# The start of a convolution and two feed-forward layers: warm-up matmuls, table load, tile 1's input and ScalarE's second high part re-ordered

## The chip, the cores and the metric

One core of a Trainium2 chip. The time is that of one launch in device microseconds (us); the median of the runs shown is the figure that the prediction is about.

## The reference, cut to what matters

```python
x = causal_conv(x, softmax(weight))   # (4, 4096, 192), 7 taps, one softmax row per head of 24 channels
h = x @ w_in                          # 16384 x 192 by 192 x 2048
x = (h * cos(h)) @ w_out              # back to 16384 x 192
h = x @ w_in2
out = (h * clip(h + 3, 0, 6) / 6) @ w_out2
```

## The kernel before, in words

The 16384 tokens are cut into 32 tiles of 512. Channels lie on partitions: 128 of them in a main part, 64 in a tail. Each tile goes through layer 1 (L1, with the cosine) and layer 2 (L2, with the clip). A layer of a tile is a **phase** of 8 **slots**, and a slot makes two chunks (halves) of 128 hidden channels. The phases run L1 of tile 0, L1 of tile 1, L2 of tile 0, L1 of tile 2, L2 of tile 1 and so on, 64 phases and 512 slots in all; slots are numbered from 0 here. The first three phases are called setup 0 (slots 0 to 7), setup 1 (8 to 15) and setup 2 (16 to 23).

Every fp32 operand is split in a high part (fp32r, a rounding copy) and a low part (the difference), and products of high by high, high by low and low by high are summed. Two independent streams of matmuls use the upper and the lower 64 rows of the array at once (`lower` and `upper`, L520 and L539). A slot has 19 turns, one matmul of each stream in a turn: 9 first products each into `h_ps` (L450), and 10 second products (L457, L464) of the slot three before it. The first three slots have nothing to mix and run 14 turns, filled up with `unread` matmuls (`alone`, L572).

What one half of a slot goes through in L1: TensorE makes `h_ps`; ScalarE copies it to an integer (L692); VectorE subtracts (`fraction`, L821); ScalarE takes the cosine (L702); VectorE multiplies (`gated`, L832), which frees the half of `h_ps` for the slot after next (the wait at L501); ScalarE copies the high part `g_hi` (`high_part`, L704); GpSimd subtracts the low part `g_lo` (L1057). In L2 ScalarE does one Relu (L694) and VectorE one operation (L835) in place of the four. Every engine executes its list in the order in which it is written, so what stands behind a wait waits too.

Beside the slots, in an order written by hand:

- **Weights** come in 18 pieces. SyncE loads them (`load_piece`, L393); the stage buffer of a piece is reloaded when the low part of the piece before it in that buffer is done (L415). The high part is copied by ScalarE (L735) or VectorE (`weight_high`, L921; which slot, HIGH_BY_DVE in L268), the low part by GpSimd (`weight_low`, L1060; LOW_IN in L273 says before which slot's g_lo).
- **Input.** A tile's four main blocks and two tail blocks are loaded by SyncE (L379 to L391), tile 2's right behind piece 11 (L413), and VectorE transposes them (`turn_main` L866, `turn_x` L871, the latter in the last slot of a phase).
- **Convolution.** VectorE does the seven taps of the main part and, from tile 2 on, of the tail, one instruction for a tap. For tiles 0 and 1 the sum of the main part is kept in PSUM (`conv_first`, L912), and TensorE does both tails with f32 matmuls by diagonals (`convolve_tails`, L655). From tile 2 on the sums are in SBUF (`conv_taps`, L926). How many taps are done by the end of which slot is in the tables of L282 to L285.

Before slot 0, TensorE warms up on ones (L649), spreads the taps over the partitions (L431), warms up again and convolves the tails; ScalarE loads the exponential table with the softmax (L780), then the sine table (L782), makes the seven diagonals, and copies the high parts of weight pieces 0 to 3, of the input, and of pieces 4 and 5 (L787 to L796). `phase` of each engine runs the slots.

## Time and profile before

| | |
|---|---|
| runs (3) | 2240.67, 2240.82, 2241.79 us; median 2240.82 |
| the profiled execution's own time | 2242.02 us |
| its span, first to last instruction | 2240.3 us |
| PE, PEld, DVE, ACT, POOL busy | 99%, 82%, 81%, 77%, 67% of the span |
| granted TensorE clock over the span | 1.00 |

The span is 1.7 us under the execution's own time. Busy shares are averages; the start differs from the rest, so the start is read by itself. Slots are told apart by the one matmul in each that reads `in_twin` (L450), the fifth of the lower stream; it starts 0.9 us behind the slot's first matmul (four turns).

### The profile page before, as it was taken

The numbers are of one execution on the slowest core, as the hardware profiler recorded it, in microseconds if no ns is written. First come the engines' busy times: TensorE is split into PE (matmuls) and PEld (weight loads), VectorE is DVE, ScalarE is ACT, GpSimd is POOL, SyncE is SP. The second block draws the span as 40 slices with busy tenths as digits, with TensorE's granted clock in tenths as the row PEclk, the third lists the DMA queues.
The fourth block names the chain that finished last, engine by engine and source line by source line (L and its number), as shares of the span: only waits on it lengthen the run. The fifth ranks groups of instructions, "written<-read, shape, count | busy, mean of one in ns | idle before, by whom it ended". The sixth has DMA issues, their size and how long they took to land.

```text
span 2240.3 us, 56720 instructions
## 1 busy us (share of the span) xinstructions
PE 2227.1 (99%) x19519; PEld 1839.8 (82%) x19519; DVE 1824.4 (81%) x2503; ACT 1732.5 (77%) x2836; POOL 1511.3 (67%) x1067
## 2 busy tenths in 40 slices
PE   8999999999999999999999999999999999999999
PEld 6888888888888888888888888888888888888887
DVE  7878888888888888888888888888888888888754
ACT  6887777887777877778777788777787777877775
POOL 6976676666666666666666666666666666666664
PEclk9999999999999999999999999999999999999999
DMA  4100000000000000000000000000000000000001
GB/s 106 50 14 16 15 0 14 14 14 14 8 6 14 14 14 14 0 14 14 14 14 1 13 14 14 14 8 6 14 14 14 14 0 14 14 14 7 3 6 23
DMA packets 208556, 33.14 MB, mean 15 GB/s; under 512 B 203136, under 2 KB 207232, under 8 KB 208512
## 3 DMA queue, kind: packets, MB, share of 16 engines
q1 hardware_dynamic: 205872, 32.20, 8.2%
q8 instruction: 30, 0.49, 0.1%
q10 hardware_dynamic: 2640, 0.33, 0.1%
q14 instruction: 14, 0.11, 0.0%
HBM read 19.92 MB, written 12.58 MB: 15 GB/s over the span
## 4 chain that ended last, share of the span: by engine, by line
PE 96%; DVE 2%; ACT 1%; issue 0%; ACTq 0%; DVEq 0%
PE h_ps L450 45%; PE acc L457 30%; PE acc_tail L464 20%; DVE gate L832 1%; ACT pre L702 1%; DVE pre L821 0%; ACT g_hi L709 0%; PE acc_tail L661 0%; ACT pre L692 0%; DVE wout L924 0%; DVE acc L909 0%; DVE in_tail L945 0%; ACT in_tail L727 0%; DVE wtail_hi L924 0%; PE acc_tail L653 0%
## 5 line engine op out<-in xcount | busy, mean ns | idle before, releaser
L1057 POOL TENSOR_TENSOR g_lo<-gate,g_hi 128x512 fp32r<-128x512 f32 x1024 | 1471.5, 1457 | 709.2 <-ACT g_hi L709 706.8
L457 PE MATMUL acc<-g_hi,wout 64*128 64x512 f32 x4096 | 1416.1, 386 | 0.0
L457 PEld LDWEIGHTS acc<-g_hi,wout 64*128 64x128 f32 x4096 | 752.9, 184 | 79.0
L450 PE MATMUL h_ps<-in_hi,win_hi 64*128 64x512 f32 x2048 | 791.7, 387 | 6.1 <-DVE gate L832 6.0
L464 PE MATMUL acc_tail<-g_lo,wout 64*128 64x512 f32 x2048 | 791.5, 386 | 0.0
L464 PE MATMUL acc_tail<-g_hi,wout 64*128 64x512 f32 x2048 | 790.8, 386 | 0.0
L450 PE MATMUL h_ps<-in_tail,wtail_hi 64*128 64x512 f32 x2048 | 790.3, 386 | 0.5 <-DVE in_tail L945 0.5
L450 PE MATMUL h_ps<-in_lo,win_hi 64*128 64x512 f32 x2048 | 790.5, 386 | 0.0
L457 PE MATMUL acc<-g_lo,wout 64*128 64x512 f32 x2048 | 790.3, 386 | 0.0
L450 PE MATMUL h_ps<-in_hi,win_lo 64*128 64x512 f32 x2048 | 790.2, 386 | 0.0
L709 ACT ACTIVATE g_hi<-gate 128x512 fp32r<-128x512 f32 x1024 | 622.4, 631 | 115.2 <-DVE gate L835 54.3
L694 ACT ACTIVATE pre<-h_ps,three 128x512 f32<-128x512 f32 x512 | 347.7, 685 | 255.9 <-PE h_ps L450 255.9
L835 DVE SCALAR_TENSOR_TENSOR gate<-pre,h_ps 128x512 f32<-128x512 f32 x512 | 338.8, 680 | 178.0 <-ACT pre L694 164.9
L821 DVE TENSOR_TENSOR pre<-pre,h_ps 128x512 f32<-128x512 int32 x512 | 338.6, 686 | 147.7 <-ACT pre L692 143.0
L450 PEld LDWEIGHTS h_ps<-in_hi,win_hi 64*128 64x128 f32 x2048 | 376.8, 184 | 51.4 <-DVE gate L832 7.6
L450 PEld LDWEIGHTS h_ps<-in_tail,wtail_hi 64*128 64x128 f32 x2048 | 376.8, 184 | 40.7 <-DVE in_tail L945 0.9
L464 PEld LDWEIGHTS acc_tail<-g_hi,wout 64*128 64x128 f32 x2048 | 376.8, 184 | 40.0 <-issue 0.3
L464 PEld LDWEIGHTS acc_tail<-g_lo,wout 64*128 64x128 f32 x2048 | 376.8, 184 | 39.7
L450 PEld LDWEIGHTS h_ps<-in_hi,win_lo 64*128 64x128 f32 x2048 | 376.9, 184 | 39.4
L457 PEld LDWEIGHTS acc<-g_lo,wout 64*128 64x128 f32 x2048 | 376.7, 184 | 39.5
L450 PEld LDWEIGHTS h_ps<-in_lo,win_hi 64*128 64x128 f32 x2048 | 376.6, 184 | 39.5
L702 ACT ACTIVATE pre<-pre,half_pi 128x512 f32<-128x512 f32 x512 | 353.4, 720 | 64.0 <-DVE pre L821 50.9
(109 smaller groups left out, 2344.9 us busy)
## 6 DMA issues: line engine op xcount, KB each, us to landing
out_dram<-o_blk SPq DMA_DIRECT2D x128, 64.0 KB, 1.8
x_in<-in_x SPq DMA_DIRECT2D x127, 64.0 KB, 2.2
blk_tail<-in_x SPq DMA_DIRECT2D x62, 64.0 KB, 2.2
out_dram<-blk_tail SPq DMA_DIRECT2D x62, 64.0 KB, 1.8
stage<-in_moe_w_out SPq DMA_DIRECT2D x7, 384.0 KB, 3.3
stage<-in_moe_w_in SPq DMA_DIRECT2D x3, 512.0 KB, 4.0
stage<-in_moe_w_in SPq DMA_DIRECT2D x6, 256.0 KB, 4.0
pre<-in_moe_w_in SPq DMA_DIRECT2D x2, 256.0 KB, 4.3
```

The source lines that it names most:

```text
L450: return pe.matmul(chunk_of(h_ps, q, half), w, x, start=start, stop=stop)
L457: return pe.matmul(acc[pair][:, :], wout[layer][rows, 2 * q + half, cols], g[rows, :], start=start, stop=stop)
L464: return pe.matmul(acc_tail[pair][:, :], wout[layer][rows, 2 * q + half, P:2 * P], g[rows, :], start=start, stop=stop)
L694: i = act.activation(p, h, ACT.Relu, bias=three[:, 0:1])
L702: act.activation(p, p, ACT.Sin, bias=half_pi[:, 0:1], scale=-TWO_PI).then_inc(cos_ready, 1)
L709: act.activation(chunk_of(g_hi, q, half), chunk_of(gate, q, half), ACT.Copy).then_inc(ghi_ready, 1)
L821: dve.tensor_tensor(p, p.bitcast(I32), chunk_of(h_ps, q, half), ALU.subtract).then_inc(frac_ready, 1)
L832: dve.tensor_tensor(g, p, h, ALU.mult).then_inc(g_ready, 1)
L835: dve.scalar_tensor_tensor(out=g, in0=p, scalar=6.0, in1=h, op0=ALU.min, op1=ALU.mult).then_inc(g_ready, 1)
L1057: pool.tensor_tensor(chunk_of(g_lo, q, half), chunk_of(gate, q, half), chunk_of(g_hi, q, half).bitcast(F32), ALU.subtract).then_inc(glo_re ...
```

## The change

- TensorE's warm-up: 5 pairs of fp32r matmuls (64 rows, 512 columns, both row halves) in place of 7 f32 ones of 128 columns; behind the spreading of the taps 3 pairs in place of 3.
- ScalarE loads the exponential table at once, with an unused activation, and then issues two main blocks (in place of one) and the two tail blocks of tile 0. Weight piece 3's high part goes behind `split_hi`.
- SyncE loads tile 1's main blocks behind pieces 0 and 1, once `xT` has been written, in place of behind piece 6.
- VectorE transposes tile 1, keeps its halo and does three of its seven taps before slot 0. In setup 0 one tap is left in slots 1 and 2 each and two in slot 3; the high parts of pieces 8 and 9, and the low tail, move by a slot.
- In setup 1 no tap of tile 2 is done; `put_halo` and all 14 taps go to setup 2, slots 16 to 20, three a slot but two in slot 19. Before, four were done in setup 1 and ten in setup 2.
- ScalarE, in setup 0 and 1: the second half's `g_hi` goes behind the two copies of the next slot.
- GpSimd's low parts of pieces 8 to 14 go one slot later.

```diff
 LAG = 3
-WARM_BEFORE = 7
+WARM_BEFORE = 5
 WARM_BEHIND = 3
...
         three = sb("three", [P, 1])
-        unused = sb("unused", [P, 1])
+        unused = sb("unused", [P, 2])
         w_soft = sb("w_soft", [H, TAPS])
...
         OUT_PIECES = {0: [5, 7, 8, 9], 2: [14, 15, 16, 17]}
-        HIGH_BY_DVE = {0: {0: 6, 1: 7, 2: 8, 4: 9, 6: 10}, 1: {0: 11, 2: 12, 4: 13, 6: 14}}
+        HIGH_BY_DVE = {0: {0: 6, 1: 7, 3: 8, 5: 9, 6: 10}, 1: {0: 11, 2: 12, 4: 13, 6: 14}}
         HIGH_IN = {2: {0: 15, 2: 16, 4: 17}}
...
         LOW_FIRST = 6
-        LOW_IN = {1: 6, 2: 7, 3: 8, 5: 9, 7: 10, 9: 11, 11: 12, 13: 13, 15: 14, 18: 15, 20: 16, 22: 17}
+        LOW_IN = {1: 6, 2: 7, 4: 8, 6: 9, 8: 10, 10: 11, 12: 12, 14: 13, 16: 14, 18: 15, 20: 16, 22: 17}
...
         LAST_TURN = DRAIN_SLOT + 1
-        CONV_FIRST = [0, 0, 1, 3, 5, 7, 7, 7, 7]
-        TURN_1 = 0
-        CONV_SECOND = [0, 0, 1, 2, 2, 2, 2, 3, 4]
+        CONV_BEFORE = 3
+        CONV_FIRST = [3, 3, 4, 5, 7, 7, 7, 7, 7]
+        CONV_SECOND = [0, 0, 0, 0, 0, 0, 0, 0, 0]
+        CONV_THIRD = [0, 3, 6, 9, 11, 14, 14, 14, 14]
         CONV = {0: [0, 0, 0, 1, 1, 1, 2, 3, 4], 1: [4, 6, 8, 10, 11, 14, 14, 14, 14]}
-        TWIN_1, TAIL_1, LOW_TAIL_1, HIGH_1, LOW_1 = 1, 3, 4, 5, 5
+        TWIN_1, TAIL_1, LOW_TAIL_1, HIGH_1, LOW_1 = 1, 2, 3, 4, 5
         LAST_LOWER = [(0, MAIN, 6), (0, TAIL, 4), (1, TAIL, 4), (1, MAIN, 6), (2, TAIL, 4), (2, MAIN, 6)]
...
-            done = {0: CONV_FIRST, 1: CONV_SECOND}.get(ph.setup, CONV[ph.layer])
+            done = {0: CONV_FIRST, 1: CONV_SECOND, 2: CONV_THIRD}.get(ph.setup, CONV[ph.layer])
             return range(done[q], done[q + 1])
...
             sp.dma_start(w_soft[:, :], weight).then_inc(w_loaded, 16)
-            load_main(0, range(P // BLK - 1))
+            load_main(0, range(2))
             for b in range(P // BLK, BLOCKS_D):
                 sp.dma_start(chip_block(x_in, o_blk_tail, b), dram_block(x_blocks, 1, b)).then_inc(x_tail_loaded, 16)
-            for n in range(LOADED_FIRST):
+            for n in range(2):
                 load_piece(n)
...
             load_main(1, range(P // BLK))
+            for n in range(2, LOADED_FIRST):
+                load_piece(n)
             for n in range(LOADED_FIRST, len(PIECES)):
...
-                ones = in_f[L2][:, 0:P]
+                ones = in_hi[L1]
                 for _ in range(count):
-                    pe.matmul(acc_tail[0][:, 0:P], ones, ones, start=True, stop=True)
+                    for rows, n in ((LOW, 0), (UP, 1)):
+                        pe.matmul(chunk_of(h_ps, n, 1), ones[rows, 0:P], ones[rows, :], start=True, stop=True)
...
-            def high_part(q, slot, reused):
+            def high_half(q, slot, half):
+                act.wait_ge(g_ready, 2 * slot + half + 1)
+                act.activation(chunk_of(g_hi, q, half), chunk_of(gate, q, half), ACT.Copy).then_inc(ghi_ready, 1)
+
+            def high_part(q, slot, reused, halves):
                 if reused:
                     act.wait_ge(mix_done, slot - G_BUFS + 1)
-                for half in range(2):
-                    act.wait_ge(g_ready, 2 * slot + half + 1)
-                    act.activation(chunk_of(g_hi, q, half), chunk_of(gate, q, half),
-                                   ACT.Copy).then_inc(ghi_ready, 1)
+                for half in range(halves):
+                    high_half(q, slot, half)
...
                         act.wait_ge(wlo_done, 2 * q + 2)
+                    if ph.setup == 2 and q == 0:
+                        high_half(SLOTS - 1, slot - 1, 1)
                     before_gate(ph.layer, q, slot)
+                    if ph.setup in (0, 1) and slot > 0:
+                        high_half((q - 1) % SLOTS, slot - 1, 1)
                     if ph.layer == L1:
...
                         split_high(L2, L1)
-                    high_part(q, slot, ph.setup != 0 or q >= G_BUFS)
+                    high_part(q, slot, ph.setup != 0 or q >= G_BUFS, 1 if ph.setup in (0, 1) else 2)
                     if splits_next(ph, q):
...
-            act.dma_start(chip_block(x_in, x_in_tail, P // BLK - 1),
-                          dram_block(x_blocks, 0, P // BLK - 1)).then_inc(x_loaded, 16)
+            act.wait_ge(const_ready, 1)
+            act.activation(unused[:, 1:2], half_pi[:, :], ACT.Exp)
+            for b in range(2, P // BLK):
+                act.dma_start(chip_block(x_in, x_in_tail, b), dram_block(x_blocks, 0, b)).then_inc(x_loaded, 16)
             for b in range(P // BLK, BLOCKS_D):
...
             act.wait_ge(const_ready, CONSTS)
-            act.activation(unused[:, :], half_pi[:, :], ACT.Sin)
+            act.activation(unused[:, 0:1], half_pi[:, :], ACT.Sin)
             act.wait_ge(taps_ready, 2)
...
                 act.activation(diagonal(t), eye, ACT.Copy, scale=taps[:, TAIL, t:t + 1]).then_inc(diag_ready, 1)
-            for n in range(4):
+            for n in range(3):
                 weight_high(n)
...
             split_hi(acc[0][:, :], L2)
+            weight_high(3)
             act.wait_ge(tails_convolved, 1)
...
                                       in_twin[L1][DT:P, :].bitcast(F32), ALU.subtract).then_inc(lo_ready[L1], 1)
-                    keep_halo(1)
                 if q == LOW_1:
...
                     if ph.convolved is not None:
-                        if ph.layer == L1 and ph.setup != 0 and q == 0:
+                        if q == 0 and (ph.setup == 2 or ph.layer == L1 and ph.setup not in (0, 1)):
                             put_halo(ph.convolved)
...
                     if ph.setup == 0:
-                        if q == TURN_1:
-                            turn_main(1)
                         split_low_1(q)
...
-            dve.memset(in_f[L2][:, 0:P], 1.0).then_inc(ones_ready, 1)
+            dve.memset(in_hi[L1][:, :].bitcast(F32), 1.0).then_inc(ones_ready, 1)
             dve.memset(half_pi[:, :], HALF_PI).then_inc(const_ready, 1)
...
                 conv_first(0, t)
-            split_low_main(acc[0][:, :], L2, 0)
-            split_low_tail(acc_tail[1][0:DT, :], L2, 0)
             keep_halo(0)
             dve.wait_ge(halo_ready, 4)
+            turn_main(1)
+            split_low_main(acc[0][:, :], L2, 0)
+            split_low_tail(acc_tail[1][0:DT, :], L2, 0)
+            keep_halo(1)
+            for t in range(CONV_BEFORE):
+                conv_first(1, t)
             phase(first_phase())
```

## Rows read from the trace of the kernel before

**Rows 1.** The page, parts 1 and 5: busy time, and the costliest group.
```profile
PE 2227.1 (99%) x19519; PEld 1839.8 (82%) x19519; DVE 1824.4 (81%) x2503; ACT 1732.5 (77%) x2836; POOL 1511.3 (67%) x1067
...
L1057 POOL TENSOR_TENSOR g_lo<-gate,g_hi 128x512 fp32r<-128x512 f32 x1024 | 1471.5, 1457 | 709.2 <-ACT g_hi L709 706.8
```

**Rows 2.** Busy time of the instructions that touch in_twin, 500 to 930.67 us.
```profile
500.00:930.67 430.67, 38.60 (x100) 18.40 (x100) 0.00 (x0) 7.58 (x12) 1.00 0.07 11
```

**Rows 3.** PE in order of time: start, us, line, tiles [idle <-releaser].
```profile
27.77 0.39 PE L450 MATMUL h_ps<-in_twin,wtail_lo 64*128 64x512 f32 x1
...
49.00 0.49 PE L450 MATMUL h_ps<-in_hi,win_hi 64*128 64x512 f32 x1 [2.65 <-DVE gate L832]
...
59.05 0.39 PE L450 MATMUL h_ps<-in_twin,wtail_lo 64*128 64x512 f32 x1
...
80.58 0.39 PE L450 MATMUL h_ps<-in_twin,wtail_lo 64*128 64x512 f32 x1
...
96.09 0.38 PE L450 MATMUL h_ps<-in_twin,wtail_lo 64*128 64x512 f32 x1
```

**Rows 4.** DVE in order of time, 20 to 70 us.
```profile
33.44 0.99 DVE L924 CAST wout<-stage 128x768 fp32r<-128x768 f32 x1
...
46.71 1.29 DVE L821 TENSOR_TENSOR pre<-pre,h_ps 128x512 f32<-128x512 int32 x2
48.26 1.30 DVE L832 TENSOR_TENSOR gate<-pre,h_ps 128x512 f32<-128x512 f32 x2 [0.26 <-ACT pre L702]
...
58.15 0.71 DVE L869 STREAM_TRANSPOSE xT<-x_in 128x512 f32<-128x512 f32 x1
```

**Rows 5.** ACT in order of time, 42 to 49 us.
```profile
42.87 1.07 ACT L692 ACTIVATE pre<-h_ps 128x512 int32<-128x512 f32 x2
47.44 1.33 ACT L702 ACTIVATE pre<-pre,half_pi 128x512 f32<-128x512 f32 x2 [3.50 <-DVE pre L821]
```

**Rows 6.** PE in order of time, the f32 convolution of the tails.
```profile
7.12 5.04 PE L661 MATMUL acc_tail<-xT_tail,oT 128*128 128x512 f32 x8
...
12.00 2.74 PE L661 MATMUL acc_tail<-xT_tail,sum_tail 128*128 128x512 f32 x6
```

**Rows 7.** SP's queue in order of time, before and with tile 1's input; the last block alone.
```profile
7.97 0.43 SPq L395 DMA_DIRECT2D gate<-in_moe_w_out  x1
...
9.64 4.44 SPq L382 DMA_DIRECT2D x_in<-in_x  x4
...
12.21 1.87 SPq L382 DMA_DIRECT2D x_in<-in_x  x1
```

**Rows 8.** DMA issues of the kernel: count, KB each, median us to landing.
```profile
gate<-in_moe_w_out SPq DMA_DIRECT2D x1, 384.0 KB, 7.6
```

**Rows 9.** ACT in order of time, the last weight part before slot 0.
```profile
17.02 0.83 ACT L738 ACTIVATE wout<-gate 128x768 fp32r<-128x768 f32 x1
```

**Rows 10.** POOL in order of time, 45 to 48 us.
```profile
45.38 1.96 POOL L1068 TENSOR_TENSOR wout<-stage,wout 128x512 fp32r<-128x512 f32 x2
```

**Rows 11.** SP's queue in order of time, 47 to 53 us.
```profile
47.37 1.11 SPq L395 DMA_DIRECT2D stage<-in_moe_w_in  x2
48.52 2.18 SPq L382 DMA_DIRECT2D x_in<-in_x  x4
50.74 1.18 SPq L390 DMA_DIRECT2D blk_tail<-in_x  x2
```

**Rows 12.** L390 from 51.5 to 51.8 us: tile 2's last block, issue and landing.
```profile
L390 SPq DMA_DIRECT2D blk_tail<-in_x x1: 488/488/488, 51.4 to 51.4; - x1
...
DMA to landing us min/median/max: 2.3/2.3/2.3
```

**Rows 13.** DVE by line and shape: count, busy us, mean ns, idle.
```profile
L909 DVE SCALAR_TENSOR_TENSOR in_ftail<-xT_tail,taps,in_ftail 64x512 f32<-64x512 f32 x180 | 288.5, 1603 | 0.0
L909 DVE SCALAR_TENSOR_TENSOR in_f<-xT,taps,in_f 128x512 f32<-128x512 f32 x180 | 226.5, 1259 | 0.0
...
L909 DVE SCALAR_TENSOR_TENSOR acc<-xT,taps,acc 128x512 f32<-128x512 f32 x12 | 9.1, 754 | 0.3
```

More of the change, by code:

```diff
@@ L1032, in _ @@
                 conv_first(0, t)
+            keep_halo(0)
+            dve.wait_ge(halo_ready, 4)
+            turn_main(1)
             split_low_main(acc[0][:, :], L2, 0)
             split_low_tail(acc_tail[1][0:DT, :], L2, 0)
-            keep_halo(0)
-            dve.wait_ge(halo_ready, 4)
+            keep_halo(1)
+            for t in range(CONV_BEFORE):
+                conv_first(1, t)
             phase(first_phase())
```

## The prediction

> **What bounds the kernel now.** The page comes first: TensorE (PE) is busy 99% of the span and GpSimd (POOL) 67% [rows 1], so the steady part can't gain from this change, which touches only the start. Next the busy time by tile: 100 of the matmuls that read `in_twin`, one per slot, in 430.67 us, so a slot takes 4.307 us [rows 2] and a turn 0.227. With that pace the order of time on PE shows what the start wastes [rows 3]. From slot 3's marker at 27.77 to slot 9's at 59.05 are 31.28 us, where six slots need 25.84: 5.44 lost, half of it in one wait of 2.65 for VectorE's gate before slot 7. From slot 14's (80.58) to slot 17's (96.09) are 15.51 where three need 12.92: 2.59 lost. Between and behind these PE runs at its pace. So some 8 us can be had in the slots, besides what lies before slot 0.
>
> Why PE waits there: half 0 of a slot is ready 12 x 0.227 + 0.39 = 3.1 us after its first matmul and half 1 after 4.25. The slot after next needs the gate of half 0 at 8.61. In L1, VectorE (DVE) needs about 2.75 us of a slot for fraction and gate (1.29, a gap of 0.26, 1.30, less overlaps) [rows 4]. Anything over 1.55 us beside them becomes a backlog. In slot 4 of before there stand two taps, a weight part, the low tail and tile 1's halo copies; ScalarE (ACT) meanwhile waits 3.50 us for the fraction [rows 5].
>
> **Start.** The exponential table goes in front, but DVE's memset of the ones is four times as wide, and ACT issues a DMA more before the softmax; I count the two as equal. The diagonals' matmuls of the tails take 5.04 us for 8, then 2.74 for 6 [rows 6]: 0.63 and 0.46 each, so TensorE comes to its upper level (2.4 GHz) on the way. Whether fp32r pairs bring it there sooner no row shows. All 14 at 0.43 would end 1.5 us sooner than 14.6, all at the lower level's 0.85 some 4.4 us later. A gain there is hidden: ACT makes the last weight part, piece 5, at 17.02 to 17.85 [rows 9], just before it copies slot 0's first half, and piece 5 lands 7.6 us after its issue [rows 8] at 7.97 [rows 7]. SyncE (SP) now issues tile 1's four blocks ahead of pieces 2 to 6. At 9.64 they took 4.44 us of SP's queue, the last alone 1.87 [rows 7]; tile 2's four took 2.18 [rows 11]. I take the nearest to the latter, 2.1 us, as few bytes are in flight then: pieces 2 to 6 are issued 2 us later, piece 5 lands at 17.6, ACT is through with it at 18.4. **+0.2** us for slot 0; ends -0.6 (the clock, no delay) and +5.6 (each block held up for 1.87, which is 5.4 more, piece 2 holding ACT's split as well). Turning tile 1 and three taps (0.71 + 3 x 0.75 [rows 4, 13]) lie in DVE's idle time before slot 0.
>
> **Setup 0.** ACT now copies the next slot before the second g_hi, about 0.55 us sooner for DVE. I walk through the slots with the durations of rows 4 and 5, from an unchanged gate 0. The turn (0.71) is out of slot 0, so gate 1 and with it slot 3 come 0.8 us sooner: at 26.0 in place of 26.8 (27.77 less four turns). Slots 1 and 2 have a tap each and piece 7: gates 2 and 3 are there at 30.25 and 34.55, in time for slots 4 and 5 (30.3, 34.6). Behind gate 3, slot 3 has two taps (1.5), piece 8 (0.99) and the low tail (0.7, as half of the 1.30 of two gates): DVE is free at 38.2, fraction to gate half 0 takes 1.55 + 0.67, so gate 4 is there at 40.4 where slot 6 is due at 38.95: **1.5 us stall**. Slot 4 has nothing beside it; slots 7, 8 and 9 start in time, at 44.8, 49.1 and 53.4. Slot 9 started at 59.05 - 0.9 = 58.15: **-4.75** us (0.8 + 5.44 - 1.5). The ends are -5.5 and -3.5 (piece 8 or 9 held up once more by as much as the 1.3 of a second POOL operation would be).
>
> **What is late next: tile 2's input.** DVE turns tile 2 in slot 7. SP loads it behind piece 11, which waits for piece 9's low part on POOL. Before: that part ends at 47.34 [rows 10], SP issues piece 11 at 47.37, the tail blocks end their issue at 51.9 [rows 11], the last one starts at 51.43 and lands 2.3 us later [rows 12]: at 53.7, 6.4 us after the low part, 4.4 us before DVE's turn at 58.15 [rows 4]. Now that low part goes a slot later, behind g_lo of slot 5 whose second half goes behind ACT's copies of slot 6: copies end 46.4, g_hi 47.0, g_lo 48.35, low part 50.3. The input is there at 56.7, DVE comes for it at 52.7. After the two transposes (57.3), fraction and gate of slot 8 end at 59.5; slot 10 is due at 57.7: **+1.85**. Ends 0 and +2.5.
>
> **Setup 1.** Here ACT splits tile 0's layer-2 input between slots 12 and 13, and DVE's weight parts remain; four taps are gone, and the copies come 0.55 sooner, against the first of the three gaps before slots 15, 16 and 17. By the same walk gate 13 is early for slot 15. The low tail, from SBUF like the slow taps, and piece 14 still cost some 0.4 at slots 16 and 17. 2.59 - 0.4: **-2.2**; ends -2.6 (all of it) and -1.2 (the 0.55 alone at each gap, and some of the taps).
>
> **Setup 2.** The fourteen taps of tile 2 now stand in slots 16 to 20. A tap that sums in SBUF has a mean of 1.26 (main) and 1.60 us (tail), one in PSUM 0.754 [rows 13]. The trace shows no other difference than POOL's work beside it, and POOL is full in these slots. Three taps are about 4.2 us, two 2.5, the gate 1.3, the drain of slot 19 another 1.3: DVE has 5.5, 5.5, 5.1 and 5.5 us in slots 17 to 20 against PE's 4.3. That is a backlog of 4.4 us; by the walk DVE comes in with some 2.3 to spare, so slots 21, 22 and 23 wait 0.2, 0.7 and 1.2: **+2.1**. Ends 0 (taps at 0.754, as in PSUM: 3.6 us a slot) and +3.8 (all at 1.60).
>
> The Trainium skill (SBUF — State Buffer, section Who interferes with whom) says that a VectorE instruction with two SBUF inputs contends with a GpSimd instruction that reads SBUF, and that the one that comes second blocks until the first ends. That speaks against the move from setup 1 to setup 2: by it, the twelve two-input taps could each wait out a whole g_lo. The means of rows 13 agree that such taps cost more, so far by half to a whole microsecond. Its worst case is a rival below.
>
> **The sum.** +0.2 - 4.75 + 1.85 - 2.2 + 2.1 = -2.8 us. The profiled execution took 2242.02 with a span of 2240.3; it would be 2239.2 and 2237.5. It stands 1.2 us over the median, so the median goes from 2240.82 to 2238.0. What a measurement of this kernel can tell from no change is about 0.2%, 4.5 us: faster means under 2236.3, slower over 2245.3.
>
> **Rivals.**
> - As summed, both new waits there: 0.48, 2238.0, its own range 2236.8 to 2239.6.
> - One of the two is absorbed (tile 2's blocks early enough, or DVE's slack in setup 2 enough): 0.20, 2236.0. For it: the slack of 4.4 us at DVE's turn before; against: the low part is a slot later.
> - Both absorbed: 0.08, 2234.1.
> - The change doesn't do what it says: g_hi's second half behind the copies feeds POOL late, so that PE waits for g_lo in slots with a low weight part. The slack that I find is 3.2 us, and such a part takes 1.96 [rows 10]; with a second delay of a POOL operation (1.457 [rows 1]) it is 0.2 to 0.4 over. Seven such slots at 0.35 give back 2.4: 0.14, 2240.4.
> - **Slower:** weights behind tile 1's blocks. If SP is held up 1.87 us at each block, piece 2 is issued 7.5 us later, ACT stands before it with `split_hi` behind, and slot 0 comes 5.6 us later in place of 0.2, with the rest as summed: 2238.0 + 5.4 = 2243.4. It decides once piece 5 lands after some 17.4 (18.2 less 0.83 [rows 9]). For it the 1.87 [rows 7], against it the 2.18 for four [rows 11] and the little in flight at 5.6 us. 0.08.
> - Each two-input tap waits out a whole POOL operation (1.457 [rows 1]): 12 x (0.75 + 1.46) = 26.5 us against my 17.8, so 8 more: 2246. 0.02. The page on SBUF named above gives the rule; the means of rows 13 are well under it.
>
> **How the numbers follow.** The range from 2234.6 to 2241.0 takes in the first four but half of the third, and leaves out the last two. Faster by over 0.2%: half of the second case, the third and a little of the first, 0.23. Slower: the last and the far end of the fifth, 0.03. Within: 0.74.
>
> **What would show it.** In the changed kernel: slot 9's marker near 54.3, slot 7 without a wait; a gap of about 1.5 us before slot 6 and of 1.9 before slot 10, there with DVE waiting for `x_in` in slot 7; no gap before slot 15; gaps before slots 21 to 23 with VectorE's taps behind one another; slot 24's marker 2.8 us earlier than before, and from there an even pace. Piece 5 landed by 17.6 and slot 0's first copy near 18.4. The forecast is wrong if slot 0's copy comes over 1 us off, if the turn of tile 2 finds its input, or if PE waits for POOL anywhere.

## The result and the profile after

| | before | after |
|---|---|---|
| median of the runs | 2241.76 us (13 runs, 2240.14 to 2242.34) | 2246.32 us (13 runs, 2245.12 to 2247.24) |
| ratio to before, 95% interval | | 1.002 [1.0012, 1.0029] |
| profiled execution's own time, span | 2242.02, 2240.3 us | 2246.53, 2244.8 us |
| granted TensorE clock over the span | 1.00 | 0.999 |

The changed kernel is 4.6 us slower, where 2.8 us less were forecast; the time lies outside the range, and the interval is clear of 1. The forecast was wrong, at two of its five terms. One run of experiment 8 took 4254.20 us at a granted clock of 0.52 over its whole span, and its ratio leaves that run out.

The slots are read by the same marker as before, the matmul that reads `in_twin`. PE in order of time in the kernel after (start, us, engine, line, operation, tiles): slots 0, 9, 10, 11, 14, 17 and 24.

```profile
19.24 0.39 PE L453 MATMUL h_ps<-in_twin,wtail_lo 64*128 64x512 f32 x1
...
57.40 0.39 PE L453 MATMUL h_ps<-in_twin,wtail_lo 64*128 64x512 f32 x1
...
65.64 0.62 PE L453 MATMUL h_ps<-in_twin,wtail_lo 64*128 64x512 f32 x1
...
71.30 0.39 PE L453 MATMUL h_ps<-in_twin,wtail_lo 64*128 64x512 f32 x1
...
84.22 0.39 PE L453 MATMUL h_ps<-in_twin,wtail_lo 64*128 64x512 f32 x1
...
97.69 0.39 PE L453 MATMUL h_ps<-in_twin,wtail_lo 64*128 64x512 f32 x1
...
130.77 0.39 PE L453 MATMUL h_ps<-in_twin,wtail_lo 64*128 64x512 f32 x1
```

Slots 9, 14 and 17 stood at 59.05, 80.58 and 96.09 before [rows 3], slot 0 at 16.48 and slot 24 at 126.26. From slot 24 on the two traces run 4.5 us apart to the end (4.51 at slot 24 and at the last slot), at the pace of [rows 2]. So all of the difference lies ahead of slot 24:

| stretch | forecast | measured (after less before) |
|---|---|---|
| before slot 0 | +0.2 | 19.24 - 16.48 = +2.76 |
| slots 0 to 9 | -4.75 | 38.16 - 42.57 = -4.41 |
| slots 9 to 11, tile 2's input late | +1.85 | 13.90 - 8.61 = +5.29 |
| slots 11 to 18 | -2.2 | -2.06 |
| slots 18 to 24 | +2.1 | +2.93 |
| sum | -2.8 | +4.51 |

**Before slot 0.** VectorE in order of time; last the reason of its wait:

```profile
7.96 0.71 DVE L893 STREAM_TRANSPOSE xT_tail<-blk_tail 128x512 f32<-128x512 f32 x1 [1.91 <-DMA blk_tail<-in_x]
```

TensorE in order of time, the f32 convolution of the tails behind that transpose:

```profile
8.73 6.20 PE L665 MATMUL acc_tail<-xT_tail,oT 128*128 128x512 f32 x8 [1.38 <-DVE xT_tail L893]
14.77 2.74 PE L665 MATMUL acc_tail<-xT_tail,sum_tail 128*128 128x512 f32 x6
```

Before, the eight began at 7.12 and took 5.04 [rows 6]. Now they begin 1.61 us later, behind a wait of 1.38, and take 1.16 more, since more of them ran at the lower clock level (a matmul each 0.85 us in place of 0.43). Together that is the difference of 2.76, to rounding. The second part scatters: in the five profiles that have this start the eight took 5.31 to 6.67, in the nine others 4.72 to 6.10, so 1.16 is this pair's number and not the change's alone. The weights are not the cause: SP's queue in order of time (start, us from first issue to the end of the last) shows tile 1's four blocks in 1.91 us, and ScalarE reached piece 5 with slot 0 already running.

```profile
5.59 1.91 SPq L383 DMA_DIRECT2D x_in<-in_x  x4
```

ScalarE in order of time, the last weight part of the start [rows 9 before: 17.02]:

```profile
19.78 0.83 ACT L744 ACTIVATE wout<-gate 128x768 fp32r<-128x768 f32 x1
```

**Slots 9 to 11.** GpSimd, SyncE, VectorE, ScalarE and TensorE in order of time: piece 9's low part, tile 2's issues, their consumer, and who stands behind it.

```profile
51.04 2.44 POOL L1082 TENSOR_TENSOR wout<-stage,wout 128x512 fp32r<-128x512 f32 x2
...
54.67 2.18 SPq L383 DMA_DIRECT2D x_in<-in_x  x4
56.89 2.41 SPq L391 DMA_DIRECT2D blk_tail<-in_x  x2
...
60.10 0.71 DVE L882 STREAM_TRANSPOSE xT<-x_in 128x512 f32<-128x512 f32 x1 [4.45 <-DMA x_in<-in_x]
61.44 0.70 DVE L888 STREAM_TRANSPOSE xT_tail<-blk_tail 64x512 f32<-64x512 f32 x1 [0.62 <-DMA blk_tail<-in_x]
...
62.75 1.33 ACT L706 ACTIVATE pre<-pre,half_pi 128x512 f32<-128x512 f32 x2 [5.12 <-DVE pre L834]
...
64.32 0.50 PE L453 MATMUL h_ps<-in_hi,win_hi 64*128 64x512 f32 x1 [3.31 <-DVE gate L845]
```

Read it downwards: the low part ends at 53.5 where it ended at 47.34 before [rows 10], the issues start at 54.67 where they started at 48.52 [rows 11], VectorE waits 4.45 and 0.62 where it came to data already there [rows 4], and behind it the cosine and then TensorE wait. TensorE's own wait isn't the whole loss. Busy time of the engines by stretch (stretch, length, busy us and count of PE, PEld, DVE, ACT, POOL, granted clock, DMA share, GB/s):

```profile
60.00:65.00 5.00, 1.69 (x16) 1.18 (x14) 4.01 (x7) 1.98 (x4) 1.34 (x1) 1.00 0.39 118
65.00:68.40 3.40, 3.40 (x20) 2.65 (x18) 2.97 (x5) 3.12 (x6) 2.74 (x2) 0.50 0.00 0
68.40:72.00 3.60, 3.60 (x34) 2.93 (x34) 1.47 (x3) 2.45 (x6) 1.74 (x2) 1.00 0.01 2
```

TensorE was busy 1.69 us of the five, and then the granted clock stood at 0.50, the lower level of 1.2 GHz, for 3.4 us: 20 matmuls, where the next line has 34. The loss of 5.29 is 3.5 us of lateness (slot 10's first matmul at 64.32, where 57.40 - 0.9 + 4.31 = 60.81 was due), and about half of 3.4 us for the clock.

**Slots 18 to 24.** VectorE in order of time: tile 2's halo and some of its taps.

```profile
99.92 1.27 DVE L908 COPY xT_tail<-halo_tail 64x6 f32<-64x6 f32 x1
...
106.03 1.77 DVE L922 SCALAR_TENSOR_TENSOR in_f<-xT,taps,in_f 128x512 f32<-128x512 f32 x1
107.73 1.78 DVE L922 SCALAR_TENSOR_TENSOR in_ftail<-xT_tail,taps,in_ftail 64x512 f32<-64x512 f32 x1
```

The four steps from slot 19 to 23 took 4.95, 5.73, 4.75 and 4.72 in place of 4.31. The pair of taps shown, beside POOL's work, took 3.5 us, and a copy of six columns, which takes 0.16 elsewhere, took 1.27.

### The profile page after: what moved, and what is told of

Read it like the earlier page. It is cut to its first block, busy times and chain, and to the rows that moved or that the text cites. A ratio compares the mean times of both kernels' runs of the same rounds, so it can differ in the third digit from the quotient of the medians.

```text
span 2244.8 us, 56713 instructions
## 1 busy us (share of the span) xinstructions
PE 2229.0 (99%) x19515; PEld 1837.4 (82%) x19515; DVE 1825.9 (81%) x2503; ACT 1729.7 (77%) x2837; POOL 1509.3 (67%) x1067
## 4 chain that ended last, share of the span: by engine, by line
PE 95%; DVE 2%; ACT 2%; DMA 0%; issue 0%; SPq 0%; POOL 0%; ACTq 0%; DVEq 0%; POOLq 0%
PE h_ps L453 45%; PE acc L460 30%; PE acc_tail L467 20%; ACT g_hi L710 1%; DVE gate L845 0%; PE acc_tail L665 0%; ACT pre L706 0%; DMA blk_tail<-in_x 0%; ACT pre L696 0%; ACT pre L698 0%; DVE pre L834 0%; DVE gate L848 0%; DVE in_f L922 0%; DVE wout L937 0%; POOL g_lo L1071 0%
## 5 line engine op out<-in xcount | busy, mean ns | idle before, releaser
L453 PEld LDWEIGHTS h_ps<-in_hi,win_hi 64*128 64x128 f32 x2048 | 377.1, 184 | 51.8 <-DVE gate L845 5.3
```

Of the source, the lines that this page charges most:

```text
L453: return pe.matmul(chunk_of(h_ps, q, half), w, x, start=start, stop=stop)
```

## The experiments

Most start from the changed kernel. A marker is the start of the `in_twin` matmul of a slot; "slot 0 to 24" is the time between two of them, which leaves out what lies before slot 0, and "slot 6 takes 4.63" is the time from slot 5's marker to slot 6's. Numbers 1 to 5 ran once each, so only their traces are argued from; their times are given for scale (the kernel before, beside the first four, took 2241.94).

**1. The start as before** (`e_start`).

```diff
-            load_main(0, range(2))
+            load_main(0, range(P // BLK - 1))
...
-            act.wait_ge(const_ready, 1)
-            act.activation(unused[:, 1:2], half_pi[:, :], ACT.Exp)
-            for b in range(2, P // BLK):
+            for b in range(P // BLK - 1, P // BLK):
```

> The changed kernel, but SyncE again issues three of tile 0's main blocks and ScalarE one and the two tail blocks, without the early exponential table. Theory A (the start is late because tile 0's last tail block, issued third on ScalarE's queue at 3.1 us, lands at 7.87 behind weight piece 0): the tail block lands by 5 us, VectorE's wait of 1.9 us for it goes, slot 0's in_twin matmul comes at 16.5 to 17.2 in place of 19.24, and slot 24's is 2 to 2.8 us earlier than in the changed kernel. Theory B (slot 0 is late because pieces 2 to 5 come behind tile 1's blocks): the tail block comes earlier, but slot 0 stays over 18.5 and slot 24 moves by under 1 us. The wait for tile 2's input stays in both.

Measured: 2243.92 us; slot 0 at 16.96, 2.3 us earlier than in the kernel after. The stall before slot 10 stays (8.35 from slot 9 to 10). So putting back the order of issue and taking out the early table wins back about 2.3 of the 2.8 us (number 10 shows that they don't cost it alone), and the start isn't why tile 2's input is late.

**2. Tile 2's input ahead of piece 9, in place of behind piece 11** (`e_x2`). The number in the edit is that of a piece and not of a slot: SyncE issues the input from 30.89 us on, in place of 54.67. Where an expectation below says that it is loaded in slot 9, this is meant.

```diff
-                if n == 12:
+                if n == 9:
                     load_x(2)
```

> The changed kernel, but SyncE loads tile 2's input ahead of piece 9 in place of behind piece 11. Theory A (the wait of 4.45 us before the turn of tile 2 costs 3.9 us at slot 10, and the fall of TensorE's clock that follows the gap 1.4 more): the step from slot 9's to slot 10's in_twin matmul falls from 8.23 to 4.3 us and the next from 5.66 to 4.3, the granted clock is 1.00 there, and slot 24's comes 4.5 to 5.3 us earlier. Rival (VectorE's backlog or GpSimd's late low parts would hold slot 10 anyway, the input is only what shows): the steps stay over 5 us, and slot 24 moves by under 3 us.

Measured: 2240.85 us, 5.5 less than the median after. Slots 10 and 11 run at the pace, and the granted clock is 1.00 there. TensorE in order of time, slots 10 and 11 of this kernel:

```profile
61.20 0.39 PE L453 MATMUL h_ps<-in_twin,wtail_lo 64*128 64x512 f32 x1
...
65.50 0.39 PE L453 MATMUL h_ps<-in_twin,wtail_lo 64*128 64x512 f32 x1
```

This one number (12 to 9) is worth the whole 5.3 us of slots 9 to 11: with the wait gone, the fall of the clock is gone too.

**3. Four taps back in setup 1** (`e_taps`).

```diff
-        CONV_SECOND = [0, 0, 0, 0, 0, 0, 0, 0, 0]
-        CONV_THIRD = [0, 3, 6, 9, 11, 14, 14, 14, 14]
+        CONV_SECOND = [0, 0, 1, 2, 2, 2, 2, 3, 4]
...
-                        if q == 0 and (ph.setup == 2 or ph.layer == L1 and ph.setup not in (0, 1)):
+                        if ph.layer == L1 and ph.setup != 0 and q == 0:
```

> The changed kernel, but four of tile 2's fourteen taps are done in slots 8 to 15 again and ten in 16 to 23. Theory A (three taps a slot put VectorE over TensorE's pace in slots 17 to 20, which costs 2.93 us at slots 20 to 23): the steps from slot 19 to 24 are all 4.3 us, slots 15 to 17 lose at most 1 us more than the 0.57 they lose in the changed kernel, so slot 24 comes 1.9 to 2.9 us earlier. Rival (the moved taps cost the same wherever they stand): slots 15 to 17 lose as much as is won, slot 24 moves by under 1 us.

Measured: 2245.36 us. Slots 20 to 24 are even at 4.31, so setup 2's loss is the moved taps' doing. But slots 16 and 17 take 5.00 and 5.91: slot 24 stands at 129.49, only 1.3 us earlier than after. The move costs 2.9 us in setup 2 and saves 1.74 in setup 1. So slot 24 moved by less than the theory had (1.9 to 2.9) and by a little more than the rival (under 1).

**4. Both high parts at once** (`e_ghi`), without the deferral of the second one.

```diff
-                    if ph.setup == 2 and q == 0:
-                        high_half(SLOTS - 1, slot - 1, 1)
...
-                    if ph.setup in (0, 1) and slot > 0:
-                        high_half((q - 1) % SLOTS, slot - 1, 1)
...
-                    high_part(q, slot, ph.setup != 0 or q >= G_BUFS, 1 if ph.setup in (0, 1) else 2)
+                    high_part(q, slot, ph.setup != 0 or q >= G_BUFS, 2)
```

> The changed kernel, but ScalarE copies both high parts of a slot before the next slot's copies, as before the change. Theory A (the reorder gives VectorE about 0.5 us a slot and so slots 3 to 9 some 1 to 2.5 us, and makes tile 2's load late by about 1 us, as piece 9's low part on GpSimd stands behind the deferred half): slots 3 to 9 lose 1 to 2.5 us more, the wait for tile 2's input is 1 to 3 us shorter, slot 11 is within 1.5 us of the changed kernel's; slots 15 to 17 lose 0.5 to 1.5 us more. Rival (the deferred half is what makes the input late): slot 11 comes 3 us or more earlier.

Measured: 2248.45 us, of which 1.0 is this execution's later start (slot 0 at 20.28: the tail block landed at 8.44 and the eight matmuls took 6.67). From slot 0 to 24 it took 112.35 against 111.53 after, and from slot 0 to 9, ahead of the stall, 38.83 against 38.16. So the deferral is worth 0.67 us there, under the 1 to 2.5 expected. The stall before slot 10 blurs the rest, so the comparison was made again in number 9.

**5. Piece 9 a slot sooner** (`e_low9`), high part in slot 4 and low part ahead of slot 5, as tile 2's input waits behind it.

```diff
-        HIGH_BY_DVE = {0: {0: 6, 1: 7, 3: 8, 5: 9, 6: 10}, 1: {0: 11, 2: 12, 4: 13, 6: 14}}
-        LOW_IN = {1: 6, 2: 7, 4: 8, 6: 9, 8: 10, 10: 11, 12: 12, 14: 13, 16: 14, 18: 15, 20: 16, 22: 17}
+        HIGH_BY_DVE = {0: {0: 6, 1: 7, 3: 8, 4: 9, 6: 10}, 1: {0: 11, 2: 12, 4: 13, 6: 14}}
+        LOW_IN = {1: 6, 2: 7, 4: 8, 5: 9, 8: 10, 10: 11, 12: 12, 14: 13, 16: 14, 18: 15, 20: 16, 22: 17}
```

> The changed kernel, but piece 9 as before the change: high part in slot 4, low part on GpSimd ahead of slot 5's g_lo. Theory A (tile 2's load waits for that low part, which went a slot later, and the order of the loads is what costs): SyncE issues piece 11 at 48.5 to 50 in place of 53.5, tile 2's last block lands by 57, VectorE waits under 1 us for it in place of 5.1, slots 10 and 11 lose nothing to 0.6 us, the granted clock stays 1.00, and slot 24 comes 4 to 5.5 us earlier. Rival (it is the deferred half of g_hi that makes the low part late, the slot matters little): piece 11 is still issued after 51.5 and slot 10's step stays over 6 us.

Measured: 2241.16 us, slot 24 at 125.28, 5.5 us earlier. VectorE comes to tile 2 without a wait, and SP has the issues out by 53.8. VectorE, then SyncE, of this kernel in order of time:

```profile
55.03 0.70 DVE L882 STREAM_TRANSPOSE xT<-x_in 128x512 f32<-128x512 f32 x1
...
50.38 2.18 SPq L383 DMA_DIRECT2D x_in<-in_x  x4
52.60 1.24 SPq L391 DMA_DIRECT2D blk_tail<-in_x  x2
```

So the chain of the forecast is the right one: low part of piece 9, piece 11, tile 2's blocks, VectorE. The two tail issues take 1.24 here, and 2.41 in the kernel after.

**6. Numbers 1 and 2 together** (`e_both`).

> Both single edits at once: tile 0's input issued as before the change (SyncE three main blocks, ScalarE one and the tails, no early table) and tile 2's input loaded ahead of piece 9. Theory A (the two losses are separate: 2.3 us at the start and 5.3 at slots 10 and 11): slot 0's in_twin matmul at 16.5 to 17.2, slot 10 and 11 at even steps, slot 24's at 122 to 123.5; the time is 7 to 8 us under the changed kernel, 2238.0 to 2239.5, faster than before the change by 2 to 4 us. Rival (what comes earlier at the start only waits later, for weights): 2240 to 2242, with new steps over 4.5 us in slots 3 to 9.

Measured: 2238.44 us median (11 runs, 2237.87 to 2239.81) against 2241.88 of the kernel before beside it (27 runs), ratio 0.9987 [0.9978, 0.9996]. Its profile is of its fastest execution (2237.87). Slot 0 at 16.29, slot 24 at 122.07, 8.7 earlier than after: 2.95 before slot 0, 5.29 in slots 9 to 11, 0.46 elsewhere. With the two failed terms taken out, the rest of the change is a gain of 3.4 us.

**7. The warm-up alone, on the kernel before** (`b_warm`).

```diff
-WARM_BEFORE = 7
+WARM_BEFORE = 5
...
-                ones = in_f[L2][:, 0:P]
+                ones = in_hi[L1]
...
-                    pe.matmul(acc_tail[0][:, 0:P], ones, ones, start=True, stop=True)
+                    for rows, n in ((LOW, 0), (UP, 1)):
+                        pe.matmul(chunk_of(h_ps, n, 1), ones[rows, 0:P], ones[rows, :], start=True, stop=True)
...
-            dve.memset(in_f[L2][:, 0:P], 1.0).then_inc(ones_ready, 1)
+            dve.memset(in_hi[L1][:, :].bitcast(F32), 1.0).then_inc(ones_ready, 1)
```

> The kernel before with the new warm-up alone: 5 and 3 pairs of fp32r matmuls of 512 columns in place of 7 and 3 f32 ones of 128. Theory A (the warm-up changes nothing that counts: in all traces so far TensorE stays at its lower level until some 10 to 15 us, long after it): within 0.5 us of before, slot 0's matmul at 16 to 17.5, the diagonals' matmuls still start at spaces of 0.85 us. Rival (the pairs bring the upper level sooner): those matmuls start at spaces of 0.43 from the first and the time is 0.7 to 1.5 us under before. Third (pairs of half the rows count as less activity, the level rises later): 0.7 us or more over before.

Measured: 2242.59 us (11 runs), ratio 1.0005 [0.9996, 1.0014]; slot 0 at 16.35 against 16.48. The pairs make no difference at slot 0 and none in the time that is clear of noise. The median is 0.7 us above the kernel before, though, outside the 0.5 of theory A and at the edge of the third rival. That rival's reason isn't what the trace shows: the eight matmuls of the tails took 4.78 us in place of 5.04, and what this profile loses, it loses at slot 8 (5.92 in place of 4.70), behind a fall of the clock.

**8. Four taps in slots 8 to 10** (`e_spread`): number 6, with ten taps left for setup 2.

```diff
-        CONV_SECOND = [0, 0, 0, 0, 0, 0, 0, 0, 0]
-        CONV_THIRD = [0, 3, 6, 9, 11, 14, 14, 14, 14]
+        CONV_SECOND = [0, 1, 3, 4, 4, 4, 4, 4, 4]
...
-                        if q == 0 and (ph.setup == 2 or ph.layer == L1 and ph.setup not in (0, 1)):
+                        if ph.layer == L1 and ph.setup != 0 and q == 0:
```

> The kernel with both edits, and the taps of tile 2 split anew: four in slots 8 to 10 (one, two, one), where VectorE has only a weight part or nothing beside the gates, ten in slots 16 to 20. Theory A (a tap is free where VectorE stays under TensorE's 4.31 us a slot, and costs where it goes over): steps from 19 to 24 all 4.3, the steps of 8 to 15 all 4.3, 16 as in the changed kernel; 2.5 to 3 us under the kernel with both edits, 2235 to 2237. Rival (a tap costs GpSimd or VectorE the same anywhere): within 1 us of it.

Measured: 2240.56 us median (11 runs, 2240.09 to 2241.66 and the one of 4254.20), ratio 0.9994 [0.9985, 1.0004], 2.1 slower than number 6. Slots 20 to 24 are even, but slots 11, 13, 15 and 16 take 6.24, 5.63, 5.45 and 5.25. Both the theory and the rival missed. What the expectation had left out is the halo: VectorE in order of time, one of its two copies of six columns, which took 1.83 and 1.26. They stand ahead of the loss at slot 11; whether they also bring the losses at slots 13 to 16 isn't shown.

```profile
57.96 1.83 DVE L905 COPY xT<-halo 128x6 f32<-128x6 f32 x1
```

**9. Number 6 without the deferral** (`e_noghi`), the edit of number 4.

> e_both without the later second high part (ScalarE makes it ahead of the next copies, as in the kernel before). Theory (the deferral pays a little in every setup slot): slots 3 to 9 take 0.7 to 1.5 us more than in e_both and slots 15 and 16 0.6 more; 0.8 to 2 us above e_both's 2238.4, so 2239.2 to 2240.4. Rival (it only moves waits): within 0.5 us of e_both.

Measured: 2240.89 us median (10 runs), ratio to before 0.9998 [0.9989, 1.0007], 2.45 above number 6. Both start within 0.04 us of one another; slots 0 to 9 take 39.23 against 37.67, and slots 15 and 16 5.15 and 5.24 against 4.31 and 4.84. By the medians the deferral is worth 2.5 us, a little more than the theory's upper end (2.46 against number 11, which has the deferral too). Of the 1.56 us in slots 0 to 9 some 0.5 is luck of number 6's profile: there VectorE's copy of weight piece 6 took 0.69 us, and slots 3 and 4 are even; in number 11, with the same list for these slots, the copy took 1.80 and slots 0 to 9 38.19. Number 6, then number 11:

```profile
21.94 0.69 DVE L935 CAST wtail_hi<-stage 128x1024 fp32r<-128x1024 f32 x1
```

```profile
21.96 1.80 DVE L937 CAST wtail_hi<-stage 128x1024 fp32r<-128x1024 f32 x1
```

**10. The order of issue alone, on the kernel before** (`b_issue`).

```diff
-            load_main(0, range(P // BLK - 1))
+            load_main(0, range(2))
...
+            act.wait_ge(const_ready, 1)
+            act.activation(unused[:, 1:2], half_pi[:, :], ACT.Exp)
+            for b in range(2, P // BLK):
```

> The kernel before with only the start's new order of issue: the exponential table first, and tile 0's two tail blocks third and fourth on ScalarE's queue in place of second on their own; warm-up, tile 1's load, taps and high parts as before. Theory (the late tail block costs the start 2 to 3 us): tile 0's last tail block lands at 7 to 8 us, the first twin group stands at 18.5 to 19.5 us in place of 16.48, and the time is 2.0 to 2.8 us above the kernel before. Rival (the block lands late only because tile 1's blocks are issued beside it): first twin group within 0.5 us of 16.48 and no change of the time.

Measured: 2241.11 us median (10 runs), ratio 0.9997 [0.9988, 1.0007], slot 0 at 16.30. My theory fell: the last tail block is third and fourth in line here too, and it is early. L780 of this kernel, the issues of tile 0's tail blocks, with DMA from issue to landing (min, median, max):

```profile
L780 ACTq DMA_DIRECT2D blk_tail<-in_x x2: 510/510/510, 2.1 to 2.7; - x2
...
DMA to landing us min/median/max: 2.5/2.6/2.6
```

The same issues in the kernel after, L790:

```profile
L790 ACTq DMA_DIRECT2D blk_tail<-in_x x2: 511/511/511, 2.5 to 3.1; - x2
...
DMA to landing us min/median/max: 2.7/3.7/4.8
```

There the last block is issued 0.43 us later, at 3.09, with SP's issue of weight piece 0 at 3.26, and takes 4.8 us in place of 2.6. This is no single case: in all five profiles of kernels in which it is issued at 3.1 it took 4.8 to 5.5 us, and in the nine in which it is issued by 2.7 it took 2.8 at most. That it waits for the weight piece behind it is likely and not shown; no run moved that piece alone. What puts it later is another edit: the memset of the ones, four times as wide for the new warm-up (0.48 us in place of 0.17), stands ahead of the memset of `half_pi`, for which ScalarE waits before the table, and its four DMA issues with it. Neither edit alone moves slot 0 later (numbers 7 and 10). That is a new theory, so it got a run.

**11. `half_pi` ahead of the ones** (`e_memset`): number 2 and two lines exchanged.

```diff
+            dve.memset(half_pi[:, :], HALF_PI).then_inc(const_ready, 1)
             dve.memset(in_hi[L1][:, :].bitcast(F32), 1.0).then_inc(ones_ready, 1)
-            dve.memset(half_pi[:, :], HALF_PI).then_inc(const_ready, 1)
```

> The changed kernel with tile 2's input loaded in slot 9 (e_x2), and besides the memset of half_pi ahead of the memset of the ones. Only the start differs from e_x2. Theory (the wide memset holds back the exponential table's wait, and with it ScalarE's four DMA issues, by 0.4 us; the last tail block is then issued 0.17 us ahead of weight piece 0 and lands with it): that block is issued near 2.65 and lands before 5.8 us, the first twin group stands 1.5 to 2.8 us earlier than e_x2's 18.81, at 16.0 to 17.3, and the time is 2238.0 to 2239.4 in place of 2240.85. Rival (issued third and fourth on ScalarE's queue, with tile 1's blocks behind it, it lands late anyway): the block still lands after 7.5 us and the time stays within 0.5 us of 2240.85.

Measured: 2238.43 us median (10 runs), ratio to before 0.9987 [0.9977, 0.9996]; 2.4 less than number 2's one run, and equal to number 6, which undoes the order of issue and the early table. L790 of this kernel:

```profile
L790 ACTq DMA_DIRECT2D blk_tail<-in_x x2: 511/511/511, 1.9 to 2.5; - x2
...
DMA to landing us min/median/max: 2.5/2.5/2.6
```

Its first marker:

```profile
16.32 0.39 PE L453 MATMUL h_ps<-in_twin,wtail_lo 64*128 64x512 f32 x1
```

So 2.5 us at slot 0 hang on whether a memset of 0.48 us stands ahead of one of 0.06.

**12. A version that beats both** (`e_best`): number 6, with tile 2's halo put in slot 9 and the low tail of setup 0 and 1 a slot later.

```diff
-        TWIN_1, TAIL_1, LOW_TAIL_1, HIGH_1, LOW_1 = 1, 2, 3, 4, 5
+        TWIN_1, TAIL_1, LOW_TAIL_1, HIGH_1, LOW_1 = 1, 2, 4, 4, 5
...
-                        if q == 0 and (ph.setup == 2 or ph.layer == L1 and ph.setup not in (0, 1)):
+                        if ph.layer == L1 and ph.setup != 0 and q == (1 if ph.setup == 1 else 0):
```

> e_both with tile 2's halo put in slot 9 in place of slot 16, and the low tail steps of the setup one slot later (position 4 in place of 3). Theory (the stalls of e_both before slots 6 and 20 to 23 come from the work that is put into those slots, on DVE's queue): the step to slot 6, 5.85 us in e_both, comes down to about 5.1, and the 2.9 us that slots 20 to 23 lose in e_both come down to about 1; 1.5 to 2.5 us faster than e_both's 2238.4, so 2235.8 to 2237.5. Rival (GpSimd's operations block DVE's taps in slots 20 to 23 whatever else stands there): slots 20 to 23 keep their stalls, at most 0.7 us faster, 2237.7 to 2238.6.

Measured: 2236.57 us median (11 runs, 2235.91 to 2237.44), ratio to before 0.9979 [0.997, 0.9988], 1.9 less than number 6 and 9.75 less than the kernel after. Slot 6 takes 4.63 in place of 5.86 (5.49 in number 11), though slots 3 and 4 take 0.8 more; number 11 has these 0.8 too, so they aren't this edit's. Slot 20 is even, and slots 21 to 23 still lose 0.7, 0.4 and 0.4. From slot 0 to 24 it took 104.01 against 105.78. Theory and rival both have a part: the halo's copies are out of setup 2 (in slot 9, with no operation of POOL beside them, they take 0.16 each), and the taps that POOL holds up, at 1.77 to 1.84 each, stay.

## Why the prediction was wrong

**Start, +0.2: failed, +2.76.** The step that failed reads "I count the two as equal": the exponential table in front against the wider memset and the DMA more. I weighed them as work on VectorE and ScalarE, and not as what stands ahead of tile 0's last tail block. That block was issued at 3.09 in place of 1.77 and landed at 7.87 in place of 4.5, VectorE waited 1.91, and TensorE began the tails 1.61 later. Numbers 7, 10 and 11 show the cause: the two edits together, neither alone. The second part, 1.16 us, is time at the lower clock level, and it scatters from one execution to the next. The forecast named a cost from the lower level (up to 4.4 us if all 14 stayed there), but a second step failed: "A gain there is hidden", behind ScalarE's piece 5. The tails weren't hidden, not even in the kernel before. There ScalarE waited 1.96 us for them, and piece 5 was through at 17.85, with slot 0 already running, while the first copy of slot 0 waited 0.38 more for TensorE:

```profile
14.78 0.59 ACT L727 ACTIVATE in_tail<-acc_tail 64x512 fp32r<-64x512 f32 x1 [1.96 <-PE acc_tail L661]
...
18.22 0.60 ACT L692 ACTIVATE pre<-h_ps 128x512 int32<-128x512 f32 x1 [0.38 <-PE h_ps L450]
```

In the kernel after the wait for them is 2.34 us:

```profile
17.55 0.59 ACT L733 ACTIVATE in_tail<-acc_tail 64x512 fp32r<-64x512 f32 x1 [2.34 <-PE acc_tail L665]
```

So whatever delays the tails delays slot 0. The delay of the weights was read rightly in size: tile 1's four blocks took 1.91 for the 2.1 taken, and the slower rival (1.87 for each) did not come.

**Setup 0, -4.75: right, -4.41.** The wait of 2.65 before slot 7 is gone, slot 7 takes 4.31. The gap before slot 6 was 1.14 for a forecast of 1.5, with 0.45 before slot 4 besides. How much of the gain is the deferral's depends on the pair that is compared: 0.67 (number 4 and the kernel after), 1.04 (numbers 9 and 11), 1.56 (numbers 9 and 6).

**Tile 2's input, +1.85: the chain right, the term mis-sized, +5.29.** The forecast had VectorE there at 52.7 and the input at 56.7, a wait of 4.0. The start's delay moved both ends by 2.8: VectorE came at 55.65, the low part ended at 53.5 (50.3 + 2.8 + 0.4). Then 6.4 us had been allowed from there to the last landing, and it took 7.9 (61.42): a tail block's issue took 1.88 where both took 1.18 before [rows 11], and its landing 2.6 for 2.3 [rows 12]. That made TensorE's lateness 3.5 in place of 1.85, and the rest, 1.8, is the fall of the clock, which the sum did not have at all. Numbers 2 and 5 take the wait away in two ways, and each gains 5.3 in slots 9 to 11. The upper end of +2.5 was too low for both reasons.

**Setup 1, -2.2: right, -2.06.** Slots 15 and 17 are even; slot 16 takes 4.84, a loss of 0.53 for 0.4.

**Setup 2, +2.1: right, +2.93, by a walk that erred both ways.** The backlog came, within the bounds, but a slot sooner: slots 20 to 23 lose 0.64, 1.42, 0.44 and 0.41 where 0, 0.2, 0.7 and 1.2 were walked. What brought it forward is the halo's copy of 1.27, for which the term had nothing; number 12 moves it, makes slot 20 even and leaves a loss of 1.6. The taps themselves came out cheaper than the 1.48 used. The rival by which each two-input tap waits out a whole POOL operation gives 2246, near the result, but by coincidence: the twelve such taps took from 0.73 to 1.78, a mean of 1.34, far under the rival's 2.21. Some are held for most of an operation and some not at all.

The Trainium skill (SBUF — State Buffer, section Who interferes with whom) says that of a VectorE instruction with two SBUF inputs and a GpSimd instruction that reads SBUF the second blocks until the first ends. This trace is in line with that for single taps, 1.77 for 0.73, while the mean of 1.34 stays well under the worst case.

**The rivals.** The two by which a new wait is absorbed fell: both waits came. The slower one, by tile 1's blocks, didn't come, as said. GpSimd fed late (2240.4) fell with number 9, and with TensorE's waits in the kernel after, from 16 to 130 us (who waited for whom: us in total, times, the longest): no matmul waited for POOL. One weight load did, for 0.76 us ahead of slot 0, while TensorE was still at the tails.

```profile
PE h_ps L453 <- DVE gate L845: 4.6, 4, 3.3
PE h_ps L453 <- DVE gate L848: 1.5, 2, 1.1
PE h_ps L453 <- DVE in_tail L958: 0.5, 1, 0.5
```

Without the two failed terms the sum of the others as measured is -4.41 - 2.06 + 2.93 = -3.5, and number 6 came out at -3.4. What was wrong was not the plan of the slots, but the two places where DMAs and a memset feed it.

## What to carry to other kernels

When an edit puts a wait ahead of a queue's DMA issues, follow that wait to the instruction that releases it and to everything in front of that: 0.3 us of memset became 2.5 us at the first slot, and two edits, neither of which moved slot 0 alone, cost this together. A load's slack is counted at its consumer, with the worst issue and landing seen, and a wait of TensorE like the 3.3 us here is priced with the slow stretch that may follow it. And a start is best tried in pieces: of five terms three were right, and two lines (number 11) turned a loss of 4.6 us into a gain of 3.4.

## What the runs showed that I had not expected

- **The clock can fall behind a gap.** Behind TensorE's wait of 3.3 us the granted clock was 0.50 for 3.4 us. At the gap before slot 7, whose profile has a wait of 2.65 both in the kernel before and in number 7, it fell in one and not in the other. Busy time by stretch, number 7, then the kernel before:

```profile
50.00:54.00 4.00, 4.00 (x24) 3.18 (x22) 3.09 (x5) 3.35 (x7) 2.26 (x2) 0.57 0.78 122
```

```profile
50.00:54.00 4.00, 3.89 (x34) 2.92 (x32) 2.99 (x5) 3.35 (x7) 2.36 (x2) 1.00 0.82 130
```

  Nothing here tells what decides it; slot 8 took 5.92 in place of 4.70.
- **The start scatters.** Numbers 6 and 12 have the same code before slot 0, and the eight f32 matmuls took 4.73 in one and 5.91 in the other, slot 0 standing at 16.29 and 17.47. One profile tells the start to about 1 us.
- **A tiny copy can cost as much as a large one.** Copies of 128 or 64 by 6 took 0.16 us alone and as much as 1.26 to 1.83 beside POOL's work.
- **One DMA issue took 1.88 us on SyncE** where the same line's other one took 0.49, and 0.6 or so before. It is no fluke: the same issue took 1.85 in number 1 and 1.90 in number 3, where the input is late too. What held it is open; no run took it apart.
